# A recurrent attention with two expert layers behind it, on one core: a table places the small weight product's pieces, and the attention's output is copied on chip by DMAs of ACT

## The reference

```python
# r, k, v, w, a, b: (4, 8, 768, 40); for each of the 4 * 8 heads, a state of 40 x 40, over t = 0..767
y[t]  = r[t] @ state
Sa    = state @ a[t]
state = state * w[t] - outer(Sa, b[t]) + outer(v[t], k[t])
# the heads side by side: x has 3072 tokens x 320
x = y.transpose(0, 2, 1, 3).reshape(3072, 320)
x = ((x @ w1) * (x @ w2) @ w3) @ w_out          # inner width 1024
x = maximum(x @ w_in, 0) ** 2 @ w_out2          # inner width 2048
```

## Time and profile before

| | |
|---|---|
| median of 3 runs | 1144.99 us (1140.64 to 1148.37) |
| the profiled execution | 1147.82 us, of which the span of the profile is 1145.3 us |
| PE busy | 1066.2 us, 93% of the span |
| PEld, DVE, ACT, POOL busy | 904.7, 634.8, 410.3, 553.3 us |
| granted TensorE clock, mean | 0.972 of full speed |
| chain that ended last | PE 82%, DVE 6%, issue 4%, ACT, DMA, SPq and POOL 2% each |
| DMAs on the output's way | 96 of 40 KB from `y_out`, 24 of 128 or 256 KB to `x_raw` |

### The profile page before, as it was taken

How to read it: one execution, slowest core, us unless ns; L and a number is a source line. 1 busy time by engine, 2 the same in 40 slices (tenths; PEclk the granted TensorE clock), 3 DMA queues, 4 the chain that set the end, 5 groups by cost and what they waited for, 6 DMA issues and landing times.

```text
span 1145.3 us, 27871 instructions
## 1 busy us (share of the span) xinstructions
PE 1066.2 (93%) x11056; PEld 904.7 (79%) x11056; DVE 634.8 (55%) x986; ACT 410.3 (36%) x763; POOL 553.3 (48%) x1579
## 2 busy tenths in 40 slices
PE   4688775899998999999999999999999999999998
PEld 4466655787787888888888889888888888887897
DVE  5344444566876755666655666555666556333343
ACT  2233322333543433444333433333444333333232
POOL 4746544726557436557535656634755653700000
PEclk9898986899999999999999999999999999999999
DMA  9342436574676864655755566565458554447552
GB/s 185 69 110 66 97 69 161 164 200 117 184 179 220 234 156 137 152 137 155 204 146 129 139 164 167 163 169 134 130 155 180 178 138 122 123 137 243 167 173 80
DMA packets 269120, 172.74 MB, mean 151 GB/s; under 512 B 201408, under 2 KB 231104, under 8 KB 268992
## 3 DMA queue, kind: packets, MB, share of 16 engines
q1 hardware_dynamic: 268992, 170.97, 57.1%
HBM read 144.18 MB, written 26.74 MB: 149 GB/s over the span
## 4 chain that ended last, share of the span: by engine, by line
PE 82%; DVE 6%; issue 4%; ACT 2%; DMA 2%; SPq 2%; POOL 2%; DVEq 0%; ACTq 0%
PE moe_bank L754 29%; PE moe_bank L818 13%; PE moe_bank L803 9%; PE both L716 4%; PE both L628 4%; PE moe_bank L788 3%; PE both L663 3%; PE both L655 2%; PE both L731 2%; PE both L727 2%; PE both L699 2%; PE both L637 2%; PE both L613 1%; PE both L707 1%; PE both L622 1%
## 5 line engine op out<-in xcount | busy, mean ns | idle before, releaser
L580 POOL TENSOR_TENSOR inv_tmp<-blk,inv 128x60 f32<-128x60 f32 (+24 forms) x744 | 242.5, 326 | 272.0 <-DVE blk L1167 215.5
L584 POOL TENSOR_TENSOR inv<-inv,inv_tmp 128x60 f32<-128x60 f32 (+24 forms) x744 | 265.0, 356 | 58.3
L818 PE MATMUL moe_bank<-v_ring,h_hi 128*128 128x320 f32 x768 | 178.1, 319 | 0.0
L754 PE MATMUL moe_bank<-xT_hi,w_ring 128*128 128x512 f32 x480 | 134.0, 409 | 10.4 <-DVE xT_lo L1250 10.4
L1245 DVE TENSOR_TENSOR hidden<-left 128x512 f32<-128x512 f32 x96 | 67.5, 703 | 128.9 <-ACT left L1011 128.9
L754 PE MATMUL moe_bank<-x2T_hi,w_ring 128*128 128x512 f32 x480 | 132.9, 406 | 0.0
L818 PEld LDWEIGHTS moe_bank<-v_ring,h_hi 128*128 128x128 f32 x768 | 127.4, 189 | 3.3
L1233 DVE TENSOR_TENSOR h_lo<-hidden,h_hi 128x512 fp32r<-128x512 f32 x144 | 99.2, 689 | 47.1 <-ACT h_hi L999 46.6
L818 PE MATMUL moe_bank<-v_ring,h_lo 128*128 128x320 f32 x384 | 119.3, 311 | 0.0
L1011 ACT ACTIVATE left<-moe_bank 128x512 f32<-128x512 f32 x96 | 57.3, 597 | 172.0 <-PE moe_bank L754 100.4
L999 ACT CAST h_hi<-hidden 128x512 fp32r<-128x512 f32 x144 | 89.4, 621 | 77.2 <-DVE hidden L1241 38.2
(11 more groups left out here) (98 smaller groups left out, 1658.0 us busy)
## 6 DMA issues: line engine op xcount, KB each, us to landing
w_ring<-gate_rows SPq DMA_DIRECT2D x40, 640.0 KB, 4.5
w_ring<-win_rows SPq DMA_DIRECT2D x40, 640.0 KB, 4.0
v_ring<-wout_rows SPq DMA_DIRECT2D x80, 320.0 KB, 2.9
v_ring<-fold_rows SPq DMA_DIRECT2D x48, 384.0 KB, 4.3
gate_rows<-w_ring SPq DMA_DIRECT2D x8, 640.0 KB, 3.4
win_rows<-w_ring SPq DMA_DIRECT2D x8, 640.0 KB, 4.1
wout_rows<-v_ring SPq DMA_DIRECT2D x16, 320.0 KB, 2.9
stage<-in_moe_w SPq DMA_DIRECT2D x8, 512.0 KB, 5.3
```

The lines of the kernel that those rows point to most:

```text
L580: nc.gpsimd.tensor_tensor(tmp, x[:, j, 0:j].unsqueeze(2).broadcast_to([P, j, X - lo]), mine[:, j:j + 1, lo:X].broadcast_to([P, j, X - lo]) ...
L584: nc.gpsimd.tensor_tensor(mine[:, 0:j, lo:X], mine[:, 0:j, lo:X], tmp, ALU.add).then_inc(solve, 1)
L754: last = nc.tensor.matmul(bank(use)[:], w, x, start=n == 0, stop=n == len(terms) - 1)
L818: last = nc.tensor.matmul(bank(f"o{s}")[:, 0:M], h[at % RING][:, s * P:(s + 1) * P], weights[:, rest * M:(rest + 1) * M], start=f == 0 and ...
```

## The change

- The pieces' slots come from three lists, `TURN_AT`, `HALF_AT` and `DONE_AT`. BEFORE, the number of slots ahead of window 0, grows from 3 to 5; the experts still begin at slot (4, 4). Of the 16 halves, six now lie in window 0, three in window 1 or, for one, at slot (2, 0), and the last four at slots (3, 3), (3, 5), (3, 9) and (3, 11).
- The DRAM tensor `xT`, `store_y` and `load_x` are gone. ACT issues the copies of a window from `y_out` straight to `x_raw`, behind `copy_state(n)` (`store_x`). A head's 40 features are cut where they cross a group of partitions, and the last 64 features go to two places, so that there are 12 DMAs for a window, 288 in all.
- Half of w_out gets a tile of its own, `wo_half`. SP loads the first w3 block ahead of w_out, and the first `uv` tiles later. ACT's splits of weights no longer wait for the whole product.

```diff
@@ -99,8 +99,8 @@
-    LEAD = 63
-    FOLD_AT = 3
+    BEFORE = 5
+    LEAD = BEFORE + 60
     LOOK = 3
@@ -157,6 +157,7 @@
         out_rows = sb("out_rows", [P, SUB, M])
+        wo_half = sb("wo_half", [P, GT // 2 * M])
@@ -218,6 +219,20 @@
             return slice(DP * q, DP if q == 0 else E)
+        def x_places(h):
+            places, e = [], 0
+            while e < D:
+                k, row = divmod(h * D + e, P)
+                count = min(D - e, (REM if k == 2 else P) - row)
+                places.append((k, row, e, count))
+                if k == 2:
+                    places.append((k, REM + row, e, count))
+                e += count
+            return places
+        Y_STORES = sum(16 * len(x_places(h)) for h in range(H))
@@ -263,7 +278,7 @@
-        wo_raw = [flat(x_raw)[:, 0:GT // 2 * M], flat(out_rows)[:, 0:GT // 2 * M]]
+        wo_raw = [wo_half[:], flat(out_rows)[:, 0:GT // 2 * M]]
         w3T = [left, hidden]
@@ -272,13 +287,15 @@
-        def fold_step(t):
-            k, idle = divmod(t - FOLD_AT, 2)
-            if k <= 0 or idle:
-                return 0, "turn" if k == 0 and not idle else None
-            ft, step = (k - 1) // 3, (k - 1) % 3
-            return (ft + 1, "turn") if step == 0 else (ft, "first" if step == 1 else "second")
+        def slot(n, at):
+            return BEFORE + 14 * n + at
+        TURN_AT = [3, 4, slot(0, 3), slot(0, 4), slot(0, 11), slot(1, 9), slot(2, 3), slot(2, 11)]
+        HALF_AT = [[slot(0, 0), slot(0, 2)], [slot(0, 3), slot(0, 4)], [slot(0, 5), slot(0, 9)],
+                   [slot(1, 3), slot(1, 5)], [slot(1, 11), slot(2, 0)], [slot(2, 5), slot(2, 9)],
+                   [slot(3, 3), slot(3, 5)], [slot(3, 9), slot(3, 11)]]
+        DONE_AT = [slot(0, 3), slot(0, 5), slot(1, 0), slot(1, 7), slot(2, 2), slot(2, 11), slot(3, 7), slot(3, 12)]
@@ -326,30 +342,6 @@
                     sp.dma_start(buffer, src).then_inc(signal, 16)
-            y_rows = xT_dram.rearrange("(x q e) (b s) -> q b e x s", q=2, e=D, b=B)
-            def store_y(n):
-                half, c = n % 2, n // 2
-                sp.wait_ge(y_scaled, n + 1)
-                for q in range(2):
-                    for y in range(2):
-                        sp.dma_start(y_rows[q][2 * half + y][:, :, c * C:(c + 1) * C],
-                                     y_out[half][half_rows(q, D), X // 2 * y:X // 2 * (y + 1), :]).then_inc(
-                                         y_stored[half], 16)
-            def load_x(i):
-                sp.wait_ge(multiplied, FT)
-                tile = xT_dram.rearrange("k (b s) -> k b s", b=B)[:, :, 2 * C * i:2 * C * (i + 1)]
-                wait(sp, x_split, i)
-                for h in range(2):
-                    sp.wait_ge(y_stored[h], 64 * 2 * (i + 1))
-                for k in range(2):
-                    sp.dma_start(x_raw[:, k, :].rearrange("p (b s) -> p b s", b=B),
-                                 tile[k * P:(k + 1) * P]).then_inc(x_loaded, 16)
-                for lo in (0, REM):
-                    sp.dma_start(x_raw[lo:lo + REM, 2, :].rearrange("p (b s) -> p b s", b=B),
-                                 tile[2 * P:M]).then_inc(x_loaded, 16)
@@ -428,15 +420,15 @@
                 for t in range(LEAD):
-                    ft, step = fold_step(t)
-                    if step == "turn" and ft < FT:
-                        sp.wait_ge(turned_w3, PARTS * (ft + 1))
-                        load_staged(ft + LOOK)
-                    if step == "second" and 0 < ft <= FT:
-                        store_fold(ft - 1)
-                        if ft == FT:
-                            for at in range(SLOTS):
-                                load_v(at)
+                    for ft in range(FT):
+                        if t == TURN_AT[ft]:
+                            sp.wait_ge(turned_w3, PARTS * (ft + 1))
+                            load_staged(ft + LOOK)
+                        if t == DONE_AT[ft]:
+                            store_fold(ft)
+                    if t == DONE_AT[-1]:
+                        for at in range(SLOTS):
+                            load_v(at)
                     yield
@@ -487,22 +479,24 @@
             begin(inputs.bk_loads(0))
-            begin(inputs.uv_loads(0))
-            load_wo()
+            load_staged(0)
             sp.wait_ge(turned_w, 1)
             begin(inputs.w_loads(1))
-            load_staged(0)
-            sp.wait_ge(turned_ar, 1)
-            begin(inputs.ar_loads(1))
+            next(beside)
+            load_wo()
             load_staged(1)
-            next(beside)
-            sp.wait_ge(turned_bk, 1)
-            begin(inputs.bk_loads(1))
             sp.wait_ge(cleared, len(clears))
                 begin(inputs.zv_loads(h))
-            begin(inputs.uv_loads(1))
+            sp.wait_ge(turned_ar, 1)
+            begin(inputs.ar_loads(1))
+            next(beside)
+            sp.wait_ge(turned_bk, 1)
+            begin(inputs.bk_loads(1))
+            next(beside)
             load_staged(2)
+            for h in range(2):
+                begin(inputs.uv_loads(h))
             next(beside)
@@ -532,10 +526,7 @@
                 next(beside)
-                store_y(n)
-                next(beside)
-                if n % 4 == 3:
-                    load_x(n // 4)
+                next(beside)
                 next(beside)
@@ -824,12 +815,12 @@
                 for t in range(LEAD):
-                    ft, step = fold_step(t)
-                    if ft < FT and step:
-                        if step == "turn":
+                    for ft in range(FT):
+                        if t == TURN_AT[ft]:
                             turn_w3(ft)
-                        else:
-                            multiply_w3(ft, int(step == "second"))
+                        for half in range(2):
+                            if t == HALF_AT[ft][half]:
+                                multiply_w3(ft, half)
                     yield
@@ -983,7 +976,6 @@
                 _, kind, at = splits[x]
-                act.wait_ge(multiplied, FT)
                 act.wait_ge(staged[(FT + x) % LOOK], staged_count[FT + x])
@@ -1010,19 +1002,31 @@
+            def store_x(n):
+                half, i, part = n % 2, n // 4, n // 2 % 2
+                act.wait_ge(y_scaled, n + 1)
+                wait(act, x_split, i)
+                x = x_raw[:].rearrange("p k (b s) -> p k b s", b=B)[:, :, 2 * half:2 * half + 2, C * part:C * (part + 1)]
+                y = y_out[half][:].rearrange("p (b g) t -> p g b t", b=2)
+                for h in range(H):
+                    for k, row, e, count in x_places(h):
+                        lo = DP * (h % 2) + e
+                        act.dma_start(x[row:row + count, k], y[lo:lo + count, h // 2]).then_inc(y_stored[half], 16)
             def round_x(i):
-                act.wait_ge(x_loaded, 64 * (i + 1))
+                for h in range(2):
+                    act.wait_ge(y_stored[h], Y_STORES * 2 * (i + 1))
                 if i:
                 for t in range(LEAD):
-                    ft, step = fold_step(t)
-                    if step == "turn" and ft < FT:
-                        copy_w3(ft)
-                    if step == "first" and 0 < ft <= FT:
-                        round_fold(ft - 1)
+                    for ft in range(FT):
+                        if t == TURN_AT[ft]:
+                            copy_w3(ft)
+                        if t == DONE_AT[ft]:
+                            round_fold(ft)
                     if t == LEAD - 1:
@@ -1109,6 +1115,7 @@
                     copy_state(n)
+                store_x(n)
                 next(beside)
@@ -1203,7 +1210,7 @@
                 dve.wait_ge(y_made, n + 1)
-                wait(dve, y_stored[n % 2], 64 * (n // 2))
+                wait(dve, y_stored[n % 2], Y_STORES * (n // 2))
                 nc.vector.tensor_tensor(y_out[n % 2][0:E], by_head(first, slice(0, E), C), decay[n % 3][0:E, :, 0:C],
```

More of the change, by code:

```diff
@@ L76, in zv_loads, with attention_with_experts @@
                  self.parity(self.v, n, q)) for q in range(2)]
-def attention_with_experts(nc, xT_dram, inputs, w1, w2, w3, w_out, w_in, w_out2, out):
+def attention_with_experts(nc, inputs, w1, w2, w3, w_out, w_in, w_out2, out):
     P, C, X, DP = 128, inputs.C, inputs.PAIRS, 64
@@ L197, in attention_with_experts @@
         v_loaded = [sem(f"v_loaded{x}") for x in range(SLOTS)]
-        x_loaded, x_rounded, x_split = sem("x_loaded"), sem("x_rounded"), sem("x_split")
+        x_rounded, x_split = sem("x_rounded"), sem("x_split")
         squared, hi_made, lo_made, h_used, out_stored = (
@@ L288, in attention_with_experts @@
                         [(23 + 2 * f, 1, FT + f) for f in range(FT2)])
-        assert LEAD + splits[0][0] > FOLD_AT + 2 * (3 * FT + 2)
         def due(t):
@@ L489, in _ @@
             begin(inputs.bk_loads(0))
-            begin(inputs.uv_loads(0))
-            load_wo()
+            load_staged(0)
```

(24 more changed lines are left out.)

## The result

The changed kernel takes 1371.12 us in the median (1369.53 to 1371.81, 4 runs), the kernel before 1143.74 us beside it. The ratio is 1.198, with a 95% interval of 1.194 to 1.203: 20% slower. The forecast was slower by 4%, at 1192 us, and the range ended at 1245.

The account below looks back on a forecast made before the run. PE was taken to bound the kernel beside the experts, with waits and a lower clock ahead of them. 54 us of waits less 7 from moved pieces gave 47, added to the median 1145: 1192 us, range 1137 to 1245.

Parts of the forecast that it names:

- The price of an issue: On ACT behind `copy_state`: 0.41 us for each of 12 DMA issues a window, bounds 0.295 and 0.64 us.
- the prediction's own formula: Beside the experts: time of issues from `copy_state`'s end less free time, over 18 window ends; 54 us, bounds 38 and 113.
- the cover of 2.1, 0.45 and 1.8 us: Free time between `copy_state` and `copy_r` at ends of windows 8, 9 and 14, hiding part of ACT's 4.5 us.
- kind of window end: Up to window 21, PE waits 12 us over five like 8, 20 over five like 9, 22 over eight like 14.
- The clock behind each wait: Rival, beside the experts: PE works 3 us at 1.2 GHz behind each of 18 waits; 27 us more, 1219 us; chance 0.14.
- the dose of the forecast: At window ends: ACT's 12 issues take 4.9 us, 4.5 us of it counted from `copy_state`'s end.
- The clock ahead of the experts: In the early windows: 1 us a window allowed for spells at the low clock, moving `make_z(4)` from 176.7 to 180.7 us.
- the case of cheap issues: Rival: ACT's issues at 0.05 us cost nothing beside the experts, first expert product 19 us earlier; 1126 us, chance 0.16.
- the 3.3 x 4 = 13 of the sum: Ahead of the experts: ACT's issues cost each bare window 3.3 us, as `turn_ar` covers 1.2 of 4.5.
- the pieces up to slot (0, 4): Ahead of window 0: two halves and two turns (6.7 us) fit beside POOL's first inversion; `make_u0(0)` stays at 46.8 us.
- The wait of `round_x` for the tile's load: Before the first expert product: the 3.04 us wait for the load from DRAM goes, product 2.5 us earlier with `rest_x`.
- SP's relief: On SP: removing four DMA issues a window and four a tile, with their waits, was put at nothing.

Follow-up runs that it names:

- the table's kernel: The kernel before with only the new slots of the pieces, the output still going by DRAM with SP's stores and loads: 1144.71 us, ratio 0.9999.

## Why the prediction was wrong

The direction, the place and the mechanism were right: 12 issues stand between `copy_state` and `copy_r`, and PE, which is hardly ever idle there, waits for them. Three sizes were off, and the first alone puts the result outside the range.

1. **The price of an issue**, taken as 0.41 us with 0.64 us as its bound, is 0.79 us. I took the row with the same source buffer as the nearest. What counts is the target: on chip the pieces take 0.79 us on ACT and 0.78 on SP, to DRAM the same pieces take 0.37 (on ACT). Twelve issues are then 9.15 us from `copy_state`'s end, and the prediction's own formula gives 18 x 9.15 - 27 = 138 us. Measured: 144.1. Added up, the cover of 2.1, 0.45 and 1.8 us came close at the on-chip doses, and fell 12 us short for 12 to DRAM:

| issues on ACT | us from `copy_state`'s end | formula | idle time gained behind the first product | busy time gained there |
|---|---|---|---|---|
| 4 to DRAM | 1.3 | 4 | 5.1 | 3.9 |
| 6 on chip | 4.5 | 54 | 55.9 | 29.0 |
| 12 to DRAM | 4.3 | 50 | 61.7 | 35.7 |
| 12 on chip | 9.15 | 138 | 144.1 | 50.3 |

(1.3 is 4 x 0.44 less 0.43; 4.3 is the 4.7 us of a window less 0.43.)

By kind of window end it did not hold. PE's mean wait in the kernel after is 7.7 us at ends like window 8's, 7.3 like 9's and 8.3 like 14's (formula: 7.1, 8.7, 7.4); with six issues it is 3.2, 2.5 and 3.6 us (formula: 2.4, 4.1, 2.7). So the cover was about 1.4, 2.0 and 0.9 us, at both doses, and the sum came out because the errors cancel: that is luck. At window 9 the reading let PE wait as soon as the three copies are late, but in the kernel before PE has other products until 456.56 us, 1.97 us behind the start of the copies:

```profile
456.56 1.40 PE L754 MATMUL moe_bank<-x2T_hi,w_ring 128*128 128x512 f32 x5
```

The 18 waits of the kernel after add up to 141.2 us. Behind windows 22 and 23, which the prediction left out because no `copy_r` follows, PE waits another 9.1 us, for `h_lo`, whose rounding stands behind the 12 issues too; its other waits are 6 us shorter than before.

2. **The clock behind each wait** was made a rival, with 27 us and a chance of 0.14. It is no rival: it came together with the waits at both doses. It cost 29.0 us at the dose of the forecast, near the rival's 27 (whose 3 us of slow work stood on no row), and 50.3 us at the real one, 1.6 and 2.8 us for each of 18 waits. The argument against it, that the stretch stays at 93% work, was an average. In the kernel after, the granted clock is 0.50 to 0.53 in the 5 us behind every one of the 18 waits. With six issues it is 0.50 to 0.71 behind 15 of them and stays at 1.00 behind three, of 2.45, 2.88 and 2.90 us: waits of this length often bring the low level, and not always.

3. **The clock ahead of the experts**, 1 us a window, was about 6 in windows 1 and 3 of the table's kernel and at most 3 in window 2 (estimates). So the pieces did not bring 7 us, and not the 19 us of the case of cheap issues: alone they bring 2.3 us up to the first product (200.86 against 203.17) and nothing measurable at the end. With all 12 issues: 27.7 us later, of which 4 x (9.15 - 1.2) = 32 are the issues, against the 3.3 x 4 = 13 of the sum. The runs bear both out: against 198.73 us with all copies on SP, the first product comes 32.1 us later with 12 on ACT, and 12.8 us later with six.

What held: `make_u0(0)` stayed where it was, so that the pieces up to slot (0, 4) cost nothing and neither w3 nor w_out came late:

```profile
47.00 0.85 PE L654 MATMUL both<-x_row,invT 32*32 32x40 f32 x32 [3.83 <-DVE invT L1180]
```

The wait of `round_x` for the tile's load is gone, as forecast; with the copies on SP the first product came 2.1 us earlier than with the load from DRAM (198.73 against 200.86). And SP's relief was worth nothing: with the copies on SP, 12 issues of 0.78 us a window in place of four of 0.37, the total rises by only 0.5%.

At the forecast's dose the kernel takes 1243 us. Had the price been right, the 1192 would still have been 51 us short: 29 us of slower work behind the first product, and 15 us ahead of it (211.5 against 196.4). These 15 are not the issues: with all copies on SP the first product is as late against the forecast without issues (198.7 against 196.4 - 13.2 = 183.2). They belong to the third point, where the clock is the likely cause.

## What to carry to other kernels

A DMA issue is work of the engine that issues it. Before it is moved onto a computing engine, count the issues times the price of the same kind of issue, the target's memory included, and read what that engine does next and who waits for it; an engine that is 36% busy has no room at the one place where its next operation is waited for. Then add the clock: over the waits here, of 3 and of 8 us in full work, PE's slower work came to 0.35 (12 issues on chip), 0.52 (six) and 0.58 (12 to DRAM) of the idle time gained.

## What the runs showed of the hardware

- An issue of an on-chip copy takes 0.78 us (SP) or 0.79 us (ACT), of the same rows and runs to DRAM 0.37 us. Within the on-chip ones, pieces of 16 and 32 rows take 0.65 us, of 8 rows 0.72, of 24 and 40 rows about 0.8. What in the target makes it dear was not found out.
- ACT's queue starts its first issue 0.06 us after the start of an operation of 0.43 us ahead of it: issues run beside the engine's arithmetic, but the arithmetic behind them waits.
- The Trainium skill, "DMA: Bandwidth & Descriptors", section "Issuing engines are not separate DMA queues", has the time to start a DMA as "usually small relative to the DMA itself". For a row of small copies the runs disagree: twelve starts were 9.5 us of ACT's time for copies of 4 to 20 KB each. The trace has no landing of these copies; the loads of 80 KB to `bk_raw` landed 3.1 us after their issue in the same trace, and beside that even one start of 0.79 us is a quarter.
